# Linear attention, routed experts and an MLP: the halves of experts 0 and 7 by column groups, two rows of tiles sent earlier, the last two tiles routed one by one

## The reference, cut to what matters

```python
def _attn_ref(r, k, v, w, u):            # B, H, S, D = 2, 8, 768, 48
    for t in range(S):
        cur = np.einsum('bhd,bhe->bhde', u[None] * kt, vt)
        y[:, :, t] = np.einsum('bhd,bhde->bhe', rt, state + cur)
        state = w[None, :, :, None] * state + np.einsum('bhd,bhe->bhde', kt, vt)

def _moe_ref(x, w_gate, w1, w2, capacity):   # N, D, E, F = 1536, 384, 8, 1024
    logits = x @ w_gate
    expert_idx = np.argmax(logits, axis=1)
    ...
    for i in range(N):
        e = expert_idx[i]
        if counts[e] < capacity:
            disp[e, counts[e]] = x[i]
    h = np.maximum(np.einsum('ecd,edf->ecf', disp, w1), 0.0)
    y = np.einsum('ecf,efd->ecd', h, w2)
    ...                                  # out[i] = gate_w[i] * y[expert, pos]

def _moe2_ref(x, w_in, w_out):           # 384 -> 2048 -> 384
    h = x @ w_in
    g = h * np.clip(h + 3.0, 0.0, 6.0) / 6.0
    return g @ w_out
```

## Time and profile before

| | us |
|---|---|
| median of three runs | 449.64 |
| the three runs | 449.29, 449.64, 455.79 |
| the profiled execution | 452.44 |
| its span, first to last instruction | 450.6 |

### The profile page before, as it was taken

The page is one execution under the profiler, slowest core; times in us unless marked ns, Lnnn a source line. Parts: engine busy times, 40 slices in busy tenths (PEclk is TensorE's granted clock), DMA queues, the critical chain, the costliest instruction groups (busy, mean ns, idle before and its releaser), DMA issues.

```text
span 450.6 us, 7399 instructions
## 1 busy us (share of the span) xinstructions
PE 423.4 (94%) x2796; PEld 361.0 (80%) x2796; DVE 248.4 (55%) x500; ACT 210.4 (47%) x483; POOL 76.1 (17%) x87
## 2 busy tenths in 40 slices
PE   6799988879899999999998999999999999999995
PEld 2788766767899999999886788887788888788883
DVE  8588896263989669669657323332323332333322
ACT  1366567525668568568556322334323334323321
POOL 5964775220110210210200000000000000000000
PEclk9699898599999999999999999999999999999999
DMA  7999992247575875875854100001000001000002
GB/s 239 284 322 333 293 291 86 89 137 279 180 268 194 300 263 188 303 250 195 277 171 168 41 0 1 0 0 71 0 1 0 1 0 71 2 0 1 0 0 76
DMA packets 28779, 60.57 MB, mean 134 GB/s; under 512 B 2420, under 2 KB 19473, under 8 KB 28738
## 3 DMA queue, kind: packets, MB, share of 16 engines
q1 hardware_dynamic: 26946, 55.30, 37.6%
q0 software_dynamic: 1792, 4.73, 2.8%
HBM read 49.77 MB, written 10.82 MB: 134 GB/s over the span
## 4 chain that ended last, share of the span: by engine, by line
PE 76%; DMA 10%; DVE 5%; ACT 2%; issue 2%; POOL 2%; SPq 1%; DVEq 0%; POOLq 0%
PE ps L1544 22%; PE ps L1546 22%; PE ps L1545 22%; DMA tm_in<-in_krv_tm 4%; PE ps L1571 4%; DMA dm_in<-in_rk_dm 3%; PE ps L1440 1%; DMA x_stage<-y_dram 1%; DMA xs_dram<-x_stage,slot 1%; PE ps L1480 1%; PE ps L1701 1%; PE ps L1507 1%; POOL rk L659 1%; PE ps L1607 1%; DVE w_lo L1122 1%
## 5 line engine op out<-in xcount | busy, mean ns | idle before, releaser
L1272 DVE SCALAR_TENSOR_TENSOR u_sb<-t_sb,ps 128x512 f32<-128x512 f32 x48 | 33.0, 688 | 121.9 <-ACT t_sb L929 121.9
L929 ACT ACTIVATE t_sb<-ps,three 128x512 f32<-128x512 f32 x48 | 33.0, 687 | 117.4 <-PE ps L1546 117.4
L1544 PE MATMUL ps<-h_hi,w_hi 128*128 128x512 f32 x144 | 57.5, 399 | 0.9 <-DVE h_lo L1278 0.7
L1546 PE MATMUL ps<-h_hi,w_lo 128*128 128x512 f32 x144 | 56.9, 395 | 0.0
L1544 PE MATMUL ps<-x_hi,win_hi 128*128 128x512 f32 x144 | 56.7, 394 | 0.0
L1545 PE MATMUL ps<-x_lo,win_hi 128*128 128x512 f32 x144 | 56.3, 391 | 0.0
L1546 PE MATMUL ps<-x_hi,win_lo 128*128 128x512 f32 x144 | 56.2, 390 | 0.0
L1545 PE MATMUL ps<-h_lo,w_hi 128*128 128x512 f32 x144 | 56.0, 389 | 0.0
L1544 PE MATMUL ps<-w_hi,h_hi 128*128 128x384 f32 (+1 forms) x128 | 43.6, 341 | 1.9 <-DVE h_lo L1151 1.8
L1546 PE MATMUL ps<-w_hi,h_lo 128*128 128x384 f32 (+1 forms) x128 | 43.0, 336 | 0.0
L1545 PE MATMUL ps<-w_lo,h_hi 128*128 128x384 f32 (+1 forms) x128 | 42.9, 335 | 0.0
(11 more groups left out here) (143 smaller groups left out, 798.9 us busy)
## 6 DMA issues: line engine op xcount, KB each, us to landing
raw<-in_w SPq DMA_DIRECT2D x14, 1536.0 KB, 8.5
tm_in<-in_krv_tm SPq DMA_DIRECT2D x12, 576.0 KB, 8.0
dm_in<-in_rk_dm SPq DMA_DIRECT2D x12, 448.0 KB, 11.1
xs_dram<-fill SPq DMA_DIRECT2D x2, 1544.0 KB, 9.9
raw_in<-in_w_in SPq DMA_DIRECT2D x8, 384.0 KB, 3.4
raw<-in_w_out SPq DMA_DIRECT2D x2, 1536.0 KB, 8.7
xg<-xs_dram SPq DMA_DIRECT2D x7, 386.0 KB, 7.2
x_stage<-y_dram SPq DMA_DIRECT2D x3, 768.0 KB, 4.7
```

The source lines that it names most:

```text
L929: nc.scalar.activation(t_sb[n % 2][:, :], ps[:, 3 + n % 3, :], ACT.Relu, bias=three[:, 0:1]).then_inc(t_done, 1)
L1272: nc.vector.scalar_tensor_tensor(out=u_sb[n % 2][:, :], in0=t_sb[n % 2][:, :], scalar=6.0, in1=ps[:, 3 + n % 3, :], op0=ALU.min, op1=ALU.m ...
L1544: mm(o, a_hi, b_hi, start=first, stop=False)
L1546: return mm(o, a_lo, b_hi, start=False, stop=last)
```

## The change

It does these things:

- GpSimd sends tiles 4 and 5 at the top of loop step n = 10, before `product(11)` and `weigh(11)`, instead of after them in steps 10 and 11.
- The six pairs of tiles become seven groups (`GROUPS`): five pairs, then tile 10 and tile 11 alone. `choose`, `place`, `sum_exp` and `send_x` go by group; `cum(5)` does tile 10, the new `cum_last` tile 11.
- In the halves, group 0 of the columns gets all three terms before group 1; its relu, turn, split and first chunk of the second product go between the products of group 1. `half_hi` and `half_lo` take a group. `keep_warm(6)` is gone. Half (7, 1)'s products no longer go inside half (7, 0).
- `first_four`: in expert 1 the first four chunks f have k outermost, and ScalarE and VectorE split w1 and x in a matching order.
- The splits of w1, w2 around these are in another order. Of w_out 4 chunks are split ahead of x2, 12 behind.
- The first block's `turn_x2` stands before the last two chunks of half (7, 1), without waiting for x2_lo in the first block, and `gate_y(7, 1)` after the x2 splits; the read of the verdict comes earlier on TensorE.

The diff, cut to its core:

```diff
+    GROUPS = [slice(2 * c, 2 * c + 2) for c in range(C - 1)] + [slice(NT - 2, NT - 1), slice(NT - 1, NT)]
+    NG = len(GROUPS)
...
             for n in range(NT):
+                if n == NT - 2:
+                    send_x(4)
+                    send_x(5)
                 if n + 1 < NT - B:
                     scale_kt(n + 1)
...
-                if n >= 6:
+                if 6 <= n < NT - 2:
                     send_x(n - 6)
-            for n in range(NT - 6, NT):
+            for n in range(6, NT):
                 send_x(n)
...
             w2_split_hi(0, 0)
             move_y(NT - 1)
+            w2_split_hi(0, 1)
             move_xt(NT - 2)
             first_x_hi(0)
+            w2_split_hi(0, 2)
             move_lg(NT - 2)
+            w2_split_hi(0, 3)
             move_xt(NT - 1)
+            w2_split_hi(0, 4)
+            sum_exp(C - 1)
             move_lg(NT - 1)
-            sum_exp(C - 1)
-            for f in range(1, FC):
-                w2_split_hi(0, f)
+            w2_split_hi(0, 5)
             half_relu(0, 0)
-            half_hi(0, 0)
+            sum_exp(C)
+            half_hi(0, 0, 0)
+            w2_split_hi(0, 6)
+            w2_split_hi(0, 7)
+            half_hi(0, 0, 1)
+            first_x_hi(1)
             gate_y(0, 0)
-            first_x_hi(1)
             half_relu(0, 1)
-            half_hi(0, 1)
-            for k in range(DC):
+            half_hi(0, 1, 0)
+            half_hi(0, 1, 1)
+            w1_split_hi(1, 0)
+            x_split_hi(1)
+            for k in range(1, DC):
                 w1_split_hi(1, k)
-            x_split_hi(1)
             in_split_hi(0)
...
-            w1_split_lo(0, 0)
+            for k in range(DC):
+                w1_split_lo(0, k)
+            place(C - 2)
             join(NT - 1)
-            place(C - 2)
             first_x_lo(0)
-            w1_split_lo(0, 1)
             choose(C - 1)
+            w2_split_lo(0, 0)
             place(C - 1)
-            w1_split_lo(0, 2)
-            for f in range(3):
+            for f in range(1, 3):
                 w2_split_lo(0, f)
+            choose(C)
+            place(C)
+            for f in range(3, 6):
+                w2_split_lo(0, f)
+            half_lo(0, 0, 0)
             half_relu(0, 0)
...
-            for f in range(FC):
+            for f in range(4):
                 wo_split_lo(f)
...
             for k in range(DC):
                 x2_split_lo(0, k)
-            for f in range(FC, F2C):
+            for f in range(4, F2C):
                 wo_split_lo(f)
...
+            def rest_of_half(e, m):
+
+                half_turn_h(e, m, 0)
+                half_first(e, m, 1, [1, 2])
+                if e > 0 and m == 0:
+                    pe.wait_ge(y_gated, 2 * e)
+                half_second(e, m, [0])
+                half_turn_h(e, m, 1)
...
             logits(NT - 2)
+            half_first(0, 0, 0, [0])
             turn_x(NT - 1)
-            half_first(0, 0, [(0, 0)])
+            half_first(0, 0, 0, [1])
+            cum(C - 1)
             logits(NT - 1)
-            half_first(0, 0, [(0, 1), (1, 0), (1, 1)])
-            cum(C - 1)
-            half_first(0, 0, [(2, 0), (2, 1)])
+            half_first(0, 0, 0, [2])
+            half_first(0, 0, 1, [0])
+            cum_last()
+            rest_of_half(0, 0)
+            half_second(0, 0, range(1, FC))
+            pe.wait_ge(slot_done, NG)
+            finish(C - 1).then_inc(counts_done, 1)
+
             pe.wait_ge(lg_moved, NT)
...
-            keep_warm(6)
-
             turn_half(1)
-            half_first(0, 1, [(0, 0), (0, 1), (1, 0), (1, 1), (2, 0), (2, 1)])
+            half_first(0, 1, 0, [0, 1, 2])
+            half_first(0, 1, 1, [0])
             pe.wait_ge(s_over, 1)
-            half_turn_h(0, 1)
+            rest_of_half(0, 1)
+            half_second(0, 1, range(1, 4))
             turn_xg(1)
-            half_second(0, 1)
+            half_second(0, 1, range(4, FC))
             for e in WHOLE:
                 expert(e)
...
+            for m in range(2):
+                half_first(LAST, m, 0, [0, 1, 2])
+                half_first(LAST, m, 1, [0])
+                rest_of_half(LAST, m)
+                if m == 0:
+                    half_second(LAST, m, range(1, FC))
+            pe.wait_ge(s_verdict, 1)
+            good = pe.value_load(flags[0:1, 0:1], min_val=0, max_val=1)
+            half_second(LAST, 1, range(1, FC - 2))
...
+            for k in range(DC):
+                turn_x2(0, k)
+            half_second(LAST, 1, range(FC - 2, FC))
```

More of the change, by code:

```diff
@@ L786, in sum_exp @@
                 act.wait_ge(below_done, c + 1)
-                for n in (2 * c, 2 * c + 1):
+                for n in range(GROUPS[c].start, GROUPS[c].stop):
                     if n > 0:
@@ L903, in _ @@
             act.wait_ge(l2_done, 2 * LAST)
-            for f in range(6):
+            for f in range(3):
                 w2_split_hi(LAST, f)
             half_relu(LAST, 0)
-            for f in range(6, FC):
+            for f in range(3, 5):
                 w2_split_hi(LAST, f)
-            half_hi(LAST, 0)
+            half_hi(LAST, 0, 0)
+            for f in range(5, FC):
+                w2_split_hi(LAST, f)
+            half_hi(LAST, 0, 1)
             in_split_hi(LAST)
@@ L912, in _ @@
             half_relu(LAST, 1)
-            half_hi(LAST, 1)
+            half_hi(LAST, 1, 0)
+            half_hi(LAST, 1, 1)
             act.wait_ge(half_l1, 8)
-            for k in range(FC):
+            for k in range(4):
                 wo_split_hi(k)
-            gate_y(LAST, 1)
             def x2_split_hi(q, k):
@@ L959, in _ @@
                 x2_split_hi(0, k)
-            for k in range(FC, F2C):
+            gate_y(LAST, 1)
+            for k in range(4, F2C):
                 wo_split_hi(k)
@@ L1065, in choose @@
             def choose(c):
-                two = slice(2 * c, 2 * c + 2)
-                dve.wait_ge(lg_moved, 2 * c + 2)
+                two, w = GROUPS[c], GROUPS[c].stop - GROUPS[c].start
+                dve.wait_ge(lg_moved, two.stop)
                 nc.vector.reduce_max(lmax[:, two], lg_sb[:, two, :], AX.X).then_inc(max_done, 1)
@@ L1532, in cum, with cum_last @@
                 add_onehots(r1, tri, 2 * c + 1).then_inc(cum_done, 1)
+            def cum_last():
+                r1 = slice(3 * E, 4 * E)
+                pe.wait_ge(onehot_done, NG)
+                pe.wait_ge(slot_done, NG - 1)
+                add_onehots(r1, ones_b, NT - 2)
+                add_onehots(r1, tri, NT - 1).then_inc(cum_done, 1)
             def finish(c):
@@ L1559, in half_first @@
                 j = halves_before(e, m)
-                for term, g in terms:
+                for term in terms:
                     if e == 0:
@@ L1609, in turn_xg, with first_four @@
                 i.then_inc(xg_turned, 1)
+            def first_four():
+                for k in range(DC):
+                    pe.wait_ge(half_h_lo, 4)
+                    pe.wait_ge(x_lo_done, k + 1)
+                    pe.wait_ge(w1_lo_done, DC + k + 1)
+                    for f in range(4):
+                        cols = slice(f * P, (f + 1) * P)
+                        i = split_product(ps[:, f, 0:MOST], w1_hi[:, k, cols], w1_lo[:, k, cols],
+                                          x_hi[:, k, 0:MOST], x_lo[:, k, 0:MOST], k == 0, k == DC - 1)
+                        if k == DC - 1:
+                            i.then_inc(l1_done, 1)
             def expert(e):
-                for f in range(FC):
+                if e == 1:
+                    first_four()
+                for f in range(4 if e == 1 else 0, FC):
                     n = l1_before(e) + f
-                    if n >= 4:
-                        pe.wait_ge(h_lo_done, n - 3)
-                    else:
-                        pe.wait_ge(half_h_lo, 4)
+                    pe.wait_ge(h_lo_done, n - 3)
                     for k in range(DC):
@@ L1709, in hidden @@
                     pe.wait_ge(in_lo_done, E)
[L1710 removed]
+                if n in (1, 2):
+                    pe.wait_ge(y_gated, 2 * LAST + n)
                 for k in range(DC):
@@ L1742, in mlp_block @@
                 project(q, F2C * q + F2C - 1, F2C - 1)
-            pe.wait_ge(s_verdict, 1)
-            good = pe.value_load(flags[0:1, 0:1], min_val=0, max_val=1)
-            for k in range(DC):
-                turn_x2(0, k)
             for q in range(NB):
```

107 lines of the change are left out of this document (49 added, 58 removed).

## The result

The changed kernel takes 448.8 us in the median where the kernel before takes 452.1 beside it: a ratio of 0.9928, 95% interval 0.9901 to 0.9956. Two further measurements of the same pair gave 0.9912 (0.9867 to 0.9957) and 0.9947 (0.9906 to 0.9989). So the change saves about 3 us of 452, where the prediction had 7.3. The sign is right, the time lies outside the range. The kernel before came out 2.4 us above the 449.64 that I had, so the ratio says it more fairly: 0.9928 measured, 442.3/449.64 = 0.9837 predicted. The profiled execution took 444.86 us, span 443.1.

What follows compares the result with a forecast made beforehand. TensorE's products fix the length of the whole experts and MLP, so only the seams could win: 4.6 + 0.6 + 1.9 + 0.2 = 7.3 us, from 449.64 to 442.3 us, range 438.3 to 446.5.

Steps and rivals of the forecast that it cites:

- Rows of tiles 4 and 5: End of the attention: sending these tiles ahead of GpSimd's last products starts them at 66.98 and 68.30, keeping 0.9 us.
- The wait of 2.8 us goes: Before turn_half(0): TensorE no longer waits for expert 0's first half to load; 0.9 of the 2.8 us are kept.
- First seam, 4.6: From the attention's end to turn_half(1): it starts at 97.0 instead of 101.61; bounds 1.5 us less, 3.7 more.
- the 95 that I had set as wrong: Sign of a wrong prediction: turn_half(1), forecast near 97.0, coming before 95 or after 99.
- DMA and TensorE side by side: Ahead of turn_half(1): DMA and TensorE together set its start, half landed at 96.8, products done at 96.6.
- Half (0, 1), 0.6: Expert 0's second half, worked by column groups: 11.35 us instead of 11.9, saving 0.6 us; bounds 0 and 1.0.
- first whole expert, 1.9: Expert 1 worked by rows of w1: its waits on w1_lo go, saving 1.9 us; bounds 0.8 and 2.0.
- Tail, +0.2: Last expert and start of the MLP: first output product at 248.6 against 248.77, saving 0.2 us; bounds -0.8 and +0.7.
- The second rival: MLP start: the clock falls after the pause at 245.5, costing 1.7 us, so 444.0 us; chance 0.20.
- The clock, row and rule: By the skill's rule the new 3 us pause in the MLP would throttle its first products; no run showed it.
- the other rival: First seam: the clock stays full, turn_half(1) comes at 93.3, 3.7 us more saved, so 438.6 us; chance 0.17.
- the four bad bounds: Unfavourable ends for first seam, half (0, 1), first whole expert and tail: 1.5, 0.6, 1.1 and 1.0 us less saved.

Runs made afterwards that it cites:

- e6: Changed kernel with eight w_out splits ahead of x2 instead of four, and the sends of tiles 4 and 5 in their old place: 447.71 us, ratio 0.9871.
- e8: The same kernel as e6, measured once more: 445.61 us, ratio 0.9870 to the kernel before.
- e5: Changed kernel with the sends of tiles 4 and 5 back in their old place, all else as changed: 448.53 us, ratio 0.9908.
- e3: Kernel before with only the sends of tiles 4 and 5 moved ahead of GpSimd's last products: 455.6 us, ratio 1.0017.
- r1: Changed kernel, nothing edited, run again for a second trace: 451.56 us.
- r3: Changed kernel, nothing edited, run again for a third trace: 449.63 us.
- e7: Changed kernel, nothing edited, run again beside other kernels on the same chip: 450.93 us, ratio 0.9947.
- e9: Changed kernel with the last two tiles routed as one pair, where tile 11 is routed in the changed kernel: 449.67 us, ratio 0.9979.
- e10: Changed kernel with half (0, 1) alone in whole tiles again instead of column groups: 447.9 us, ratio 0.9903.
- e4: Changed kernel with the first whole expert as before: no first_four, all of w1 split before x: 450.98 us, ratio 1.003.

## Why the prediction was wrong

**Rows of tiles 4 and 5.** Their times came out to 0.1 us. The step that failed is "The wait of 2.8 us goes ... Of 2.8 us 0.9 are kept": the wait belongs to executions whose attention ends early, as the profiled one, e6 and e8; the other three with the old sends had no wait to lose. And where it was there the seam was no longer for it. Undone in e5 and made alone in e3, the move shows no gain.

**First seam, 4.6.** Measured 3.8 at equal low clock, inside the bounds, with a standard error of 0.6. The 4.6 held the 0.9 of the sends; the 3.7 without them agree. The last send was at 88.16 instead of 90.5; in this execution the clock was back at 80.4, not near 90.5. turn_half(1) came at 94.40, below the 95 that I had set as wrong, and in r1, r3 and e7 at 102.58, 99.94 and 98.38, two of them above the 99 that I had set as wrong on the other side: a single time on this axis says little. "DMA and TensorE side by side" was right: the half lands 0.6 to 0.8 us before TensorE needs it, and e9 shows that one send more in the burst makes the DMA late. What I missed is that the first seam takes 29.7 to 37.8 us in the kernels with the change, most of the difference going with the clock.

**Half (0, 1), 0.6, and first whole expert, 1.9.** Together 2.0 us in place of 2.5; alone 0.5 (e10) and 2.1 (e4). In addition the old order's waits on w_lo bring half clock with them in some executions, a gain of 1.6 us there that I had not counted. The carrying through the whole experts was right: 85.0 us from the turn_xg of expert 2 to that of expert 7 before, 85.0 to 85.4 with the change.

**Tail, +0.2.** This is the step that failed most: -1.5 us (243.4 on the mean of four traces against 241.9 on that of three). I had the row for it ("VectorE 12 x 0.48 = 5.7 us where 3.83 stood"), and gate_y of half (7, 0) came 2.0 us sooner after the last turn_xg, against 2.1 predicted. But of these 2.0 us only 0.9 reached the x2 transposes. The load of x_stage took 5.43 instead of 4.53 us; with the 0.13 more of the y rows that is 1.0 of the missing 1.1. I had taken 0.5 for it. (In r3 the two were 3.1 and 4.55 us, about as much in sum.) With 1.9 us more of splits in the queue the first output product came 0.4 us later than before on the mean of four traces, not 0.2 sooner. The other 1.1 us lie between it and the end, and they are the clock: with half clock behind the pause the products take 198.0 us, without it 196.4, and three of the four traces have it, which makes 1.2 us on the mean; behind the last product it is 0.1 us less than before. The second rival (chance 0.20, 1.7 us) has thus come true in these three, at the place that it named, at a price of 1.5 us; in r3 it has not.

**The clock, row and rule.** The rows bear out that the long pause ahead of the MLP's output products mostly brings the clock down: a pause of 2.7 to 2.8 us was followed by half clock in six of eight traces, one of 1.83 us in none of one, 0.6 to 0.8 us in none of seven. The section "HAM oscillation" of the Trainium skill's "TensorE: Matmul & The Clock Gate" says that a wait between bursts of products throttles the engine, so that the next burst starts cold. Six of the eight traces agree; in the other two, r3 and e9, the clock stayed full behind the same pause. In the first seam the rule explains less: in the third trace of before the clock fell at 78.8, with TensorE busy all through 77 to 79 and no wait for the half; in e8 it fell at 74.4, before that wait. So the other rival, full clock through the seam, had no ground in the pause. The profiled execution came near it all the same: with full clock from 80.4 on, turn_half(1) stood at 94.40, where this rival had 93.3.

**The sum.** 3.8 + 2.0 - 1.5 = 4.3 us, and up to 0.8 more on average for the clock at w_lo, against 7.3: 0.8 are missing in the first seam, 0.5 in the two next steps, 1.7 in the tail. The ratios say 2.4 to 4.0 us, less than the pieces. These are from few traces of either order, and where the rest goes stays open; a difference of a microsecond is what their clock leaves open. The upper end of the range, 446.5, was too low by its own working: it is 442.3 and the four bad bounds (1.5 + 0.6 + 1.1 + 1.0 = 4.2), without the rival that its sentence names beside them; with the 1.7 of the second rival it would be 448.2.

## What to carry to other kernels

Before a wait is priced, look whether it is in more than one execution: an event whose two releasers are within a few microseconds of each other changes hands from one execution to the next (here the wait was in three of six), and taking it away need not shorten the stretch. When transposes are brought forward in front of the last products, count what both elementwise engines must still do behind them: here each split left behind x_lo was 0.48 us of TensorE's pause, and a long pause can take the clock with it, at 1.5 us for 3.4 us of half clock. Where the clock differs between executions, compare stretches between equal events, with the low time in each beside it, rather than whole times; and end the last stretch at the last product, since the 4.8 to 6.1 us behind it vary by as much as what is looked for.

## What the hardware showed that I had not expected

- The spread of 8 to 12 us between executions of one kernel goes with the place and the amount of half clock: 3.4 us in the seam gave 32.5 us and 20.5 us gave 39.4 in one and the same kernel (before).
- In the MLP 3.4 us of half clock cost 1.5 us, and traces without it agree within 0.15 us over 196 us of products.
- Half clock costs the seam 0.42 us per microsecond, a little under the 0.5 of work that is TensorE's alone, although this stretch is full of short transposes, routing and DMAs.
- A pair of pauses of 1.1 and 0.6 us on w_lo (1.22 and 0.18 in e4) went with a fall of the clock in three of five traces, while the 1.83 us in the MLP did not. The length of one pause alone does not decide.
